# Gated linear attention and two mixture layers on one core: scores by head over half the partitions, gate columns summed on TensorE, unread products on TensorE

## What is computed

```
for t in range(S):                      # stage 1: per head
    m_new = maximum(f[t] + m, i[t])
    f_stab, i_stab = exp(f[t] + m - m_new), exp(i[t] - m_new)
    C = f_stab * C + i_stab * outer(v[t], k[t]);  n = f_stab * n + i_stab * k[t]
    y[t] = sigmoid(o[t]) * (C @ q[t]) / maximum(abs(n . q[t]), 1)
x = y as rows of 1536 tokens x 320
logits = x @ w_gate + log1p(exp(x @ w_noise)) * noise        # stage 2: top 2 of 8
x = sum over the 2 best experts of weight * (relu(x @ w1[e]) @ w2[e])
x = sum over 4 experts of p[e] * (relu(x @ w1[e]) @ w2[e])    # stage 3
```

## Time and profile before

| | |
|---|---|
| median of three runs | 735.81 us (734.17 to 736.21) |
| the profiled execution | 737.39 us, its span 735.6 us |
| TensorE busy over the span | 675.1 us, 92% |
| its weight loads | 613.4 us |
| VectorE, ScalarE, GpSimd busy | 399.7, 286.7, 100.6 us |
| stage 1 | about the first 90 us |
| one inner pair of heads | 8.46 us |
| clock granted to TensorE, mean | 0.968 |

### The profile page before, as it was taken

How to read it: one execution, slowest core, us unless ns; L and a number is a source line. 1 busy time by engine, 2 the same in 40 slices (tenths; PEclk the granted TensorE clock), 3 DMA queues, 4 the chain that set the end, 5 groups by cost and what they waited for, 6 DMA issues and landing times.

```text
span 735.6 us, 11126 instructions
## 1 busy us (share of the span) xinstructions
PE 675.1 (92%) x4064; PEld 613.4 (83%) x4065; DVE 399.7 (54%) x667; ACT 286.7 (39%) x470; POOL 100.6 (14%) x138
## 2 busy tenths in 40 slices
PE   2999967899999999899279999999999999999997
PEld 2898825799899899899278999898898888988896
DVE  7577668756545455455246546546544554454422
ACT  6644530455444454454134334333333342332311
POOL 5343301430120220200331000201200001000000
PEclk9999886999999999999779999999999999999999
DMA  8566662376545457940276234344352333422001
GB/s 219 138 145 153 186 176 81 106 213 166 161 133 157 137 163 222 354 130 0 83 226 169 76 102 126 98 127 122 108 154 60 100 114 107 130 85 73 0 0 36
DMA packets 32855, 94.44 MB, mean 128 GB/s; under 512 B 4880, under 2 KB 14864, under 8 KB 32816
## 3 DMA queue, kind: packets, MB, share of 16 engines
q1 hardware_dynamic: 25328, 77.54, 36.4%
q0 software_dynamic: 3264, 11.15, 5.3%
q10 hardware_dynamic: 4224, 5.24, 2.0%
HBM read 79.49 MB, written 14.42 MB: 128 GB/s over the span
## 4 chain that ended last, share of the span: by engine, by line
PE 85%; DVE 6%; issue 4%; DMA 1%; ACT 1%; ACTq 0%; POOL 0%; DVEq 0%; POOLq 0%
PE pY L1148 12%; PE pY L1150 12%; PE pY L1149 12%; PE pH L1133 9%; PE pH L1134 8%; PE pH L1135 8%; PE pH L1138 4%; PE pH L1140 4%; PE psS L977 3%; PE psYa L1030 3%; PE pT L1110 2%; PE psYa L1043 1%; PE psF L1064 1%; PE pH L1092 1%; DVE h_lo L849 1%
## 5 line engine op out<-in xcount | busy, mean ns | idle before, releaser
L577 ACT ACTIVATE h_hi<-pH 128x512 fp32r<-128x512 f32 x160 | 95.7, 598 | 280.4 <-PE pH L1140 275.5
L849 DVE SCALAR_TENSOR_TENSOR h_lo<-pH,h_hi 128x512 fp32r<-128x512 f32 x160 | 110.5, 691 | 166.1 <-ACT h_hi L577 162.1
L1148 PE MATMUL pY<-w_hi,h_hi 128*128 128x320 f32 x608 | 189.9, 312 | 6.1 <-DVE h_lo L849 5.7
L1150 PE MATMUL pY<-w_hi,h_lo 128*128 128x320 f32 x608 | 187.9, 309 | 0.0
L1149 PE MATMUL pY<-w_lo,h_hi 128*128 128x320 f32 x608 | 187.8, 309 | 0.0
L1133 PE MATMUL pH<-x_hi,w_hi 128*128 128x512 f32 (+3 forms) x324 | 124.1, 383 | 8.2 <-issue 5.7
L1148 PEld LDWEIGHTS pY<-w_hi,h_hi 128*128 128x128 f32 x608 | 114.3, 188 | 15.0 <-issue 10.3
L1134 PE MATMUL pH<-x_lo,w_hi 128*128 128x512 f32 (+3 forms) x324 | 121.3, 374 | 0.0
L685 DVE TENSOR_TENSOR w_lo<-stage,w_hi 128x1024 fp32r<-128x1024 f32 (+1 forms) x79 | 107.1, 1356 | 25.4 <-ACT w_hi L523 24.4
L1135 PE MATMUL pH<-x_hi,w_lo 128*128 128x512 f32 (+3 forms) x324 | 120.8, 373 | 0.0
L1149 PEld LDWEIGHTS pY<-w_lo,h_hi 128*128 128x128 f32 x608 | 114.3, 188 | 3.1
(11 more groups left out here) (222 smaller groups left out, 633.2 us busy)
## 6 DMA issues: line engine op xcount, KB each, us to landing
stage<-in_w SPq DMA_DIRECT2D x40, 640.0 KB, 4.0
stage<-in_w SPq DMA_DIRECT2D x40, 512.0 KB, 3.6
stage<-in_w SPq DMA_DIRECT2D x40, 256.0 KB, 3.8
results_by_slot<-acc ACTq DMA_DIRECT2D x8, 640.0 KB, 3.5
results_by_slot<-X SPq DMA_DIRECT2D x8, 640.0 KB
qk<-in_qk_t SPq DMA_DIRECT2D x16, 240.0 KB
kv<-in_kv_n SPq DMA_DIRECT2D x8, 480.0 KB
og<-in_o_n SPq DMA_DIRECT2D x2, 960.0 KB, 9.1
```

Source lines behind the costliest of these rows:

```text
L577: act.activation(HH[s % 2][:, :], pH[s % 2][:, :], ACT.Relu).then_inc(hh_done[layer], 1)
L849: dve.scalar_tensor_tensor(out=HL[s % 2][:, :], in0=pH[s % 2][:, :], scalar=0.0, in1=f32(HH[s % 2][:, :]), op0=ALU.max, op1=ALU.subtract). ...
L1148: pe.matmul(y[:, 0:XD], hh, wh, start=(f == 0), stop=False)
L1150: return pe.matmul(y[:, 0:XD], hl, wh, start=False, stop=(f == NF - 1))
```

## The change

Scores: `qz`, its fills and its loads go. A head's scores are six products over its own 64 partitions, with 128 columns each, heads in turn; `psS` is laid out by head, so that the two heads of a turn write different banks, and one wait (`s_mid`) guards the bank they share. Gate columns: `er` and its two operations go. TensorE adds three products per chunk in PSUM instead, of `ig` with the identity and of `mrow` and `dc` with its negative (`minus`). GpSimd fills `decay_rows` and `carry_rows`. On ScalarE the exponentials of head 0 of pair 0 come ahead of the exponential and copy of the carries, and the value copy of pair 0 ahead of both; on VectorE and TensorE the work on the carries of pair 0 moves behind the first multiplication and the first values. Unread products (`unread`) are put on TensorE at five places: nine, four and three around the gate columns, ten after the first scores, five in the last pair in the place of the decays. The fetch counts of a pair go from 80 to 48 (three transfers), wherever they are waited for.

```diff
@@ gpsimd
             for n in range(2):
                 pool.memset(v1[n][:, :, :, D:D1], 1.0)
-            pool.memset(qz[1][:, :, :, :], 0.0).then_inc(pads, 1)
-            pool.memset(qk[1][:, :, :], 0.0).then_inc(pads, 1)
+            pool.memset(minus[:, :], 0.0).then_inc(minus_built, 1)
...
+            for tile in (decay_rows, carry_rows):
+                pool.memset(f32(tile[:, :]), 0.0).then_inc(rows_zero, 1)
+            pool.memset(qk[1][:, :, :], 0.0).then_inc(pads, 1)
@@ scalar
             act.activation(decay_rows[0:BH, :], dc[:, :], ACT.Copy).then_inc(decay_hi, 1)
-            act.wait_ge(carry_sum, 1)
-            act.activation(gr[:, :], gr[:, :], ACT.Exp).then_inc(carry_ready, 1)
-            act.wait_ge(carry_ready, 1)
-            act.activation(carry_rows[0:BH, :], gr[:, :], ACT.Copy).then_inc(carry_hi, 1)
...
+            values_in(0, 0)
+            act.wait_ge(acol_ready, 1)
             for i in range(PAIRS):
...
                     ins.then_inc(exp_done, 1)
+                    if i == 0 and h == 0:
+                        act.wait_ge(carry_sum, 1)
+                        act.activation(gr[:, :], gr[:, :], ACT.Exp).then_inc(carry_ready, 1)
+                        act.wait_ge(carry_ready, 1)
+                        act.activation(carry_rows[0:BH, :], gr[:, :], ACT.Copy).then_inc(carry_hi, 1)
@@ vector
-            dve.memset(qz[0][:, :, :, :], 0.0).then_inc(pads_qz, 1)
-            for tile in (decay_rows, carry_rows):
-                dve.memset(f32(tile[:, :]), 0.0).then_inc(rows_zero, 1)
...
-            link(dve.tensor_tensor(er[:, :], ig[:, :], mrow[:, :], ALU.subtract))
...
-            dve.tensor_tensor(er[:, :], er[:, :], dc[:, :], ALU.subtract).then_inc(acol_ready, 1)
...
                 mults(i, 0, par)
+                if i == 0:
+                    carries_split()
                 carried(i, par)
@@ tensor
+            def unread(n, bank):
+
+                for _ in range(n):
+                    pe.matmul(bank, pick_wide[:, 0:2, :].rearrange("p n d -> p (n d)"), pick_wide[:, 0:512 // HB, :].rearrange("p n d -> p (n d)"),
+                              start=True, stop=True, skip_group_check=True)
+
+            def columns(rows, one, first=False):
+                for c in range(CH):
+                    ins = pe.matmul(psM[:, c * BH:(c + 1) * BH], rows[:, c * P:(c + 1) * P], one, start=(first and c == 0), stop=True, skip_group_check=True)
+                return ins
...
+                def score(h, n):
+                    r, t = slice(h * HB, (h + 1) * HB), slice(n * P, (n + 1) * P)
+                    return pe.matmul(psS[:, h, n, :], kT[par][r, t], qT[par][r, t], start=True, stop=True, skip_group_check=True)
+
                 for c in range(CH):
-                    ins = pe.matmul(psS[:, c].rearrange("p h t -> p (h t)"), kT[par][:, c * P:(c + 1) * P],
-                                    qz[par][:, c].rearrange("p h t -> p (h t)"), start=True, stop=True, skip_group_check=True)
+                    n = (c + 4) % CH
+                    ins = score(0, n)
+                    if n == CH - 1:
+                        ins.then_inc(s_mid, 1)
+                    n = (c + 2) % CH
+                    if n == 0:
+                        pe.wait_ge(s_mid, i + 1)
+                    ins = score(1, n)
                 ins.then_inc(s_mm, 1)
...
                 values(i, 0, par)
+                if i == 0:
+                    ends()
+                    carries(0)
+                    increments(0, 0)
                 if i + 1 < PAIRS:
                     decays(i + 1)
+                else:
+                    unread(5, last_decays)
                 values(i, 1, par)
```

More of the change, by code:

```diff
@@ L118, in build @@
         iotaP = sb("iotaP", [P, P], BF16)
+        minus = sb("minus", [BH, BH])
         in_gates, in_o, in_router = sem("in_gates"), [sem(f"in_o{n}") for n in range(2)], sem("in_router")
@@ L160, in build @@
         qT, kT = ([t[:, n, :] for t in qk] for n in range(2))
-        qz = [sb(f"qz{n}", [P, CH, 2, P], F32, att) for n in range(2)]
         qg = [sb(f"qg{n}", [P, S], F32, att) for n in range(2)]
@@ L177, in build @@
         yt = sb("yt", [P, CH, 2, D], F32, att)
-        ig, fg, mrow, dd, er, dc, gr, reset = (
-            sb(n, [BH, S], F32, att) for n in ("ig", "fg", "mrow", "dd", "er", "dc", "gr", "reset"))
+        ig, fg, mrow, dd, dc, gr, reset = (
+            sb(n, [BH, S], F32, att) for n in ("ig", "fg", "mrow", "dd", "dc", "gr", "reset"))
         first = sb("first", [BH, CH], F32, att)
@@ L523, in split_hi, with values_in @@
                         act.activation(hi, src, ACT.Copy).then_inc(wh_done[layer], 1)
-            act.wait_ge(acol_ready, 2)
-            for i in range(PAIRS):
-                par = i % 2
-                act.wait_ge(qk_in[par], 80 * (i // 2) + 80)
+            def values_in(i, par):
+                act.wait_ge(qk_in[par], 48 * (i // 2) + 48)
                 if i >= 2:
@@ L531, in _ @@
                 act.activation(v1[par][:, :, :, 0:D], kv[par][:, :, 1, :, :], ACT.Copy).then_inc(v1_done, 1)
+            values_in(0, 0)
+            act.wait_ge(acol_ready, 1)
+            for i in range(PAIRS):
+                par = i % 2
+                if i >= 1:
+                    values_in(i, par)
                 act.wait_ge(decay_mm, i + 1)
@@ L688, in carried @@
             def carried(i, par):
[L689 removed]
+                dve.wait_ge(qk_in[par], 48 * (i // 2) + 48)
                 dve.wait_ge(carry_mm, i + 1)
@@ L971, in scores @@
+            columns(ig, ident[0:BH, 0:BH], first=True)
+            pe.wait_ge(gate_chain, 1)
+            columns(mrow, minus[:, :])
+            unread(4, last_decays)
+            pe.wait_ge(decay_ready, 1)
+            columns(dc, minus[:, :]).then_inc(acol_mm, 1)
+            unread(3, last_decays)
             def scores(i, par):
-                pe.wait_ge(qk_in[par], 80 * (i // 2) + 80)
+                pe.wait_ge(qk_in[par], 48 * (i // 2) + 48)
                 if i >= 1:
                     pe.wait_ge(pm_done, 2 * i)
+                def score(h, n):
+                    r, t = slice(h * HB, (h + 1) * HB), slice(n * P, (n + 1) * P)
+                    return pe.matmul(psS[:, h, n, :], kT[par][r, t], qT[par][r, t], start=True, stop=True, skip_group_check=True)
@@ L1002, in _, with ends @@
             scores(0, 0)
-            pe.wait_ge(carry_lo, 1)
-            pe.wait_ge(state_zero, 1)
-            for i in range(PAIRS):
-                who = pick_wide[:, 2 * i:2 * i + 2, :].rearrange("p h d -> p (h d)")
-                ins = pe.matmul(psC[:, 2 * CH * D1 - (PAIRS - i) * CH:2 * CH * D1 - (PAIRS - i - 1) * CH], who, carry_rows[:, P - 1:S:P], start=True, stop=True, skip_group_check=True)
-            ins.then_inc(ends_mm, 1)
-            carries(0)
+            pe.wait_ge(acol_ready, 1)
+            unread(10, psY[:, :])
+            def ends():
+                pe.wait_ge(carry_lo, 1)
+                pe.wait_ge(state_zero, 1)
+                for i in range(PAIRS):
+                    who = pick_wide[:, 2 * i:2 * i + 2, :].rearrange("p h d -> p (h d)")
+                    ins = pe.matmul(psC[:, 2 * CH * D1 - (PAIRS - i) * CH:2 * CH * D1 - (PAIRS - i - 1) * CH], who, carry_rows[:, P - 1:S:P], start=True, stop=True, skip_group_check=True)
+                ins.then_inc(ends_mm, 1)
             def increments(i, par):
@@ L1031, in values @@
                               start=(c + h == 0), stop=False, skip_group_check=True)
-            increments(0, 0)
             for i in range(PAIRS):
```

43 lines of the change are left out of this document (22 added, 21 removed).

## The result

The changed kernel takes 743.75 us (median of four runs, 742.71 to 744.64), the kernel before beside it 736.01 (734.17 to 737.41): ratio 1.0106, 95% interval 1.008 to 1.0132. It is 7.7 us slower, where I had forecast 5.4 us faster, and outside my range. (In the later sets of runs the kernel before, run beside the others, had medians of 735.92, 736.17 and 736.01, so medians of different sets can be compared to a few tenths.) The profiled execution took 743.98 us, its span is 742.2 against 735.6.

The account below looks back on a forecast made before the run. TensorE's stream of work was taken to set the pair, VectorE close behind, and VectorE's gate work the start. First pair 0.4, scores 3.7, last pair 1.3 gave 5.4 us less: 730.4 us against the median, range 727.8 to 736.4.

Parts of the forecast that it names:

- The walk of TensorE's queue, the term of the first pair: Before the first decays: gate columns and unread products let decays end at 14.1 instead of 15.75; first pair gains 0.4 us.
- slow columns: Rival, front of the stage: gate columns at ordinary load pitch, first pair loses 1.6 us, total 732.4 us; chance 0.20.
- From the decays' end on: First pair, from the end of its decays to the end of its state products: 12.95 us.
- falling inside: Rival: the clock falls inside the pairs, 4.1 us for a pair at half clock, total 738.6 us; chance 0.13.
- The gate chain on VectorE and the table load: Before the first pair: scan at 3.3, decays' low part ready at 11.4 instead of 13.99; Exp table load, 1.28 us, on path.
- Scores: Inner pairs: heads side by side, scores about 1.3 us instead of 2.63; VectorE limits the gain to 3.7 us over seven pairs.
- The last pair: Last pair: five unread products hold the clock, saving 2.3 us and costing 1.0, so 1.3 us gained.
- Everything behind moves as it is: After the attention stage: all moves forward unchanged, with perhaps some tenths where the clock rises near 122 us.
- The sum: Whole kernel: 0.4 + 3.7 + 1.3 = 5.4 us less, 732.0 against the profiled execution, 730.4 against the median.

Follow-up runs that it names:

- transposes again: The changed kernel with er and six transposes in place of the gate columns, all unread products kept: 736.70 us, ratio 1.0018.
- the old order: The changed kernel with the work on the carries of pair 0 back ahead of the first exponentials and first values: 741.38 us, ratio 1.0056.
- the version without columns: Kernel before with scores by head, GpSimd fills, and unread products (nineteen ahead of the transposes, six, one, five); transposes and carries' place kept: 728.89 us, again 729.81.
- scores alone: The kernel before with only the scores by head, padded copies of q, their fills and loads gone: 736.92 us, ratio 1.0011.
- six beside the short scores: The kernel before with only the scores by head, plus six unread products of 512 columns behind the first scores: 733.57 us, ratio 0.9986.
- the last pair without its five: The changed kernel without the five unread products in the last pair: 745.90 us, ratio 1.0131.
- the gate columns out, once more: The changed kernel with pair 0's carries in their former place, er and six transposes for gate columns, nineteen unread products in one run ahead: 732.44 us, ratio 0.9937.

## Why the prediction was wrong, point by point

**The walk of TensorE's queue, the term of the first pair.** Mis-sized, and the step that failed. I took the pitch of the transposes of the same shape (0.118 us at half clock) for the columns, and put the ordinary loads' 0.225 aside as the rival "slow columns", with 0.20, because shape and few moving columns were the same. But the instructions are not transposes: at half clock six transposes took 0.79 us in "transposes again", the twelve instructions of a set of columns 2.74. The columns measure 0.22, so the rejected bound was the right one: 36 x 0.22 is 7.9 us of queue where I had 3.3. The Trainium skill (TensorE: Matmul & The Clock Gate, LDWEIGHTS) speaks for that bound, and the trace agrees: loads of 128 columns from 16 rows take 0.22 us an instruction at half clock, those from 128 rows 0.225. But my rival had 16.1 for the decays' end, 2.0 more than my 14.1; measured were 21.2. The other 5 us are the clock, for which I had taken the recovery in the last pair (6.4 us of dense work) and assumed that it would hold once up. In the changed kernel's trace it wasn't up before 24 us; "the old order" shows it up near 9 and down again behind two sets of columns, with no gap. The four and three unread products did not hold it, and at half clock each costs 0.5. Some 3 of the 5 us hang on the execution: in three traces with the same queue the decays begin at 16.8.

**From the decays' end on.** Working: 12.95 at full clock; measured 16.1, 3.1 more, for a clock that falls at 31 us. I had this fall as the rival "falling inside", 4.1 us a pair, but gave it 0.13 and placed the cause in the inner pairs' idle half microsecond. In this trace the inner pairs hold it and the two behind the start do not; in the first of the version without columns the third and fourth lose it. The new order is not what made it ("the old order": it falls too), nor the columns ("transposes again"); what does is open. The state products of the first pair so end 9.9 us later, where I had forecast 0.4 earlier.

**The gate chain on VectorE and the table load.** Right: scan at 3.27 (3.3), low part ready at 11.4 (11.4), the load on the path with 1.28. Right and worth nothing, since TensorE's queue was later by 8.3 us. I should have read my own order: TensorE's queue ended after VectorE in every case that I worked out.

**Scores.** Right in kind, low in size. Heads do work side by side: 24 instructions in 1.54 us, not 2.8. The Trainium skill (TensorEngine Tiling (Array Packing), Key Properties) has tiles run in parallel, and 1.54 agrees; of its drain at a change of tiling mode no row shows a gap (scores run from 54.33 to 55.87, carries from 55.87, and the next state products, 60.97 + 1.15, end where the next scores begin). VectorE is the next limit, as said. 3.3 us came back in the five pairs from the third to the seventh, 0.67 each, where I had 0.53. What I left out is that in pair 0 the scores are at half clock, as the first decays' 1.62 us said, and are the long dense stretch in which the clock rose (at 20 us). In the trace of "scores alone" pair 0 ends 3.0 us later than before; the runs of "six beside the short scores" speak for the missing stretch as the reason, and do not show it.

**The last pair.** The size was right: the last spacing shrank by 1.14 us and the transposes' end by 0.56, 1.7 in all against 1.3. So was the reason, the clock held by the five: "the last pair without its five" seems to deny it by its own trace (8.19), and the thirteen traces together bear it out (before the last pair ends, the clock falls in all five without them and in none of the eight with them).

**Everything behind moves as it is.** Wrong by 1 to 3 us: the pause at 140 us. No rival of mine had it. Added instructions count even when nothing waits for them.

**The sum.** The forecast was -5.4 us (0.4, 3.7 and 1.3 gained). In the trace, first pair +9.9, second +0.75, five inner pairs -3.3, last pair and transposes -1.7, the pause and what follows +1.0 net at the end: +6.6.

## What to carry to other kernels

Walk the queue of the engine that executes in order with the slow price of each unknown instruction, and compare its end with that of the chain it is meant to shorten; a sum that TensorE makes with many thin products is not free because VectorE was the chain. Before a dense stretch is shortened or thin products are put ahead of it, look where the granted clock stands at that place: a part that gains in every steady pair can lose the same in the one pair that starts cold, so measure each part alone. One trace is one execution: where the moment of a rise or fall of the clock differs between executions, compare the runs too, and look in the trace whether the fall came before or behind what was added. Of the filler tried here, sixteen products between thin ones lost time (4 us by the medians), and the kernels with nineteen in one run up to the transposes were the fastest; those nineteen were not measured by themselves.

## What the runs showed of the hardware

The granted clock fell from 2.4 to 1.2 GHz with TensorE shown busy without a gap, behind 24 instructions of 16 columns in 3.0 us, in the midst of four dense ones ("the old order", about 12.2 us). A gap of 1.46 us behind dense work kept 2.4 GHz; it was lost in one of 2.3 us in "transposes again" and with one of 3.45 us in "the gate columns out, once more" (decays 0.97, 1.48 and 1.65 us).

Fp32 products in turn on the lower and the upper 64 rows of the array ran side by side: 1.54 us for twelve of 128 columns at full clock, 2.93 at half, where the kernel before took 2.63 for the same columns.

Twenty-nine tiny products (58 entries) in a place where TensorE had nothing to do made it wait 3.7 us later in the program. In thirteen traces the place of this wait goes by the number of added entries, divided by 256.
